# Block means of the first batch's values on TensorE instead of VectorE, and the fourth task's value products ahead of the next scores

## What is computed

```python
block, window = (32, 16)
k_sum = k.reshape(B, H, nb, block, D).max(axis=3)
v_sum = v.reshape(B, H, nb, block, D).mean(axis=3)
scores_l = scale * np.matmul(q, k.transpose(0, 1, 3, 2))      # kept where |i - j| < window
scores_s = scale * np.einsum('bhsd,bhnd->bhsn', q, k_sum) + np.log(block)
a = softmax(concatenate([scores_l_masked, scores_s]))
out = np.matmul(a, concatenate([v, v_sum]))
```

## Time and profile before

| | |
|---|---|
| time, median of 3 runs | 730.56 us (728.78 to 730.85) |
| the profiled execution | 730.36 us, its span 728.6 us |
| mean granted TensorE clock | 0.992 |
| busy: PE, DVE, ACT, POOL | 704.6, 404.5, 281.3, 66.8 us |
| DMA | 139.36 MB, mean 191 GB/s |

### The profile page before, as it was taken

One profiled execution on the slowest core, in us unless ns is written; L12 is line 12 of the kernel. 1 busy time (PEld: TensorE's weight loads), 2 busy tenths in 40 slices (PEclk: granted clock), 3 DMA queues, 4 the chain that ended last, 5 costly groups with the idle time before them and its releaser, 6 DMA issues.

```text
span 728.6 us, 12342 instructions
## 1 busy us (share of the span) xinstructions
PE 704.6 (97%) x4499; PEld 580.9 (80%) x4500; DVE 404.5 (56%) x1042; ACT 281.3 (39%) x653; POOL 66.8 (9%) x97
## 2 busy tenths in 40 slices
PE   5699999999999999999999999999999999899997
PEld 5578898898989889988988998899899884444444
DVE  4987584552795684754756364466447217453441
ACT  3745364451345433631621451064036113342430
POOL 2612000000000000000000000100100003323221
PEclk9999999999999999999999999999999999999999
DMA  9885632120708817613976739124530996699900
GB/s 206 217 196 117 133 82 55 41 48 4 286 5 326 331 60 287 285 64 103 417 301 276 261 115 367 51 103 186 219 115 10 377 348 232 243 393 396 370 3 22
DMA packets 92384, 139.36 MB, mean 191 GB/s; under 512 B 55172, under 2 KB 55456, under 8 KB 90656
## 3 DMA queue, kind: packets, MB, share of 16 engines
q1 hardware_dynamic: 89664, 133.89, 52.9%
q0 software_dynamic: 2656, 4.66, 1.9%
HBM read 104.05 MB, written 34.98 MB: 191 GB/s over the span
## 4 chain that ended last, share of the span: by engine, by line
PE 91%; DVE 4%; issue 1%; DMA 1%; ACT 1%; POOL 0%; DVEq 0%; SPq 0%; POOLq 0%
PE ps L1727 15%; PE ps L1729 15%; PE ps L1728 15%; PE ps L1977 8%; PE ps L1978 8%; PE ps L1979 8%; PE ps L2088 6%; PE ps L2116 6%; PE ps L1789 2%; PE ps L1761 2%; PE ps L1920 1%; PE ps L1775 1%; PE ps L2101 1%; PE ps L1740 1%; PE ps L1909 1%
## 5 line engine op out<-in xcount | busy, mean ns | idle before, releaser
L1977 PE MATMUL ps<-xt_hi,wb_hi 128*128 128x384 f32 x336 | 112.8, 336 | 0.0
L1979 PE MATMUL ps<-xt_hi,wb_lo 128*128 128x384 f32 x336 | 112.4, 334 | 0.0
L1978 PE MATMUL ps<-xt_lo,wb_hi 128*128 128x384 f32 x336 | 112.3, 334 | 0.0
L966 ACT ACTIVATE h_raw<-ps 128x384 f32<-128x384 f32 x96 | 47.1, 490 | 116.0 <-PE ps L1979 113.8
L1728 PE MATMUL ps<-v_lo_acc,hb_hi 128*128 128x512 f32 x216 | 84.2, 390 | 0.0
L1360 DVE SCALAR_TENSOR_TENSOR acc<-ps,dp,acc 128x512 f32<-128x512 f32 x36 | 27.0, 750 | 99.3 <-PE ps L1729 99.3
L1345 DVE TENSOR_TENSOR h_raw<-ps,h_raw 128x384 f32<-128x384 f32 x96 | 49.7, 552 | 44.4 <-PE ps L1979 44.3
L972 ACT ACTIVATE hb_hi<-h_raw 128x384 fp32r<-128x384 f32 x96 | 49.0, 525 | 52.5 <-DVE h_raw L1345 52.5
L1977 PEld LDWEIGHTS ps<-xt_hi,wb_hi 128*128 128x128 f32 x336 | 63.1, 188 | 0.4
L1978 PEld LDWEIGHTS ps<-xt_lo,wb_hi 128*128 128x128 f32 x336 | 63.1, 188 | 0.3
L1979 PEld LDWEIGHTS ps<-xt_hi,wb_lo 128*128 128x128 f32 x336 | 63.1, 188 | 0.0
(11 more groups left out here) (268 smaller groups left out, 1302.8 us busy)
## 6 DMA issues: line engine op xcount, KB each, us to landing
sets<-in_moe_w SPq DMA_DIRECT2D x72, 512.0 KB
w_aside<-wb_hi SPq DMA_DIRECT2D x3, 3584.0 KB, 17.0
w_aside<-wb_lo SPq DMA_DIRECT2D x3, 3584.0 KB, 24.8
wb_hi<-w_aside SPq DMA_DIRECT2D x21, 512.0 KB, 10.9
wb_lo<-w_aside SPq DMA_DIRECT2D x21, 512.0 KB, 11.7
acc<-in_moe_w SPq DMA_DIRECT2D x12, 768.0 KB, 5.2
w_raw<-in_moe_w SPq DMA_DIRECT2D x12, 512.0 KB, 5.5
stage<-in_k SPq DMA_DIRECT2D x16, 192.0 KB, 4.2
```

What stands on the lines that cost most here:

```text
L966: nc.scalar.activation(h_raw[:, f, half * GT:(half + 1) * GT], ps[:, bank, 0:GT], ACT.Copy).then_inc(put_by, 1)
L1977: mm(to, wb_hi[w], hi(c), start=(c == 0 and not onto), stop=False, skip_group_check=onto)
L1978: mm(to, wb_hi[w], lo(c), start=False, stop=False, skip_group_check=onto)
L1979: last = mm(to, wb_lo[w], hi(c), start=False, stop=(c == HALF_D - 1), skip_group_check=onto)
```

## The change

The four means of each block row of the first batch (`sum_values(0)` and `(1)` on DVE) are no longer made by additions. The values of the first batch are loaded in another layout (`load_early`: partition p holds positions 6p to 6p + 5 of each head, four DMAs of 192 KB in place of one of 768 KB) into the region of a later tensor, and PE multiplies six 128 x 32 matrices of 1/32 and 0 (`in_block`, made by POOL with a memset and two selections) with them (`block_means`, six products of 256 columns into 32 rows of PSUM bank 3). ACT copies the 24 x 256 means out (`copy_means`), and turn(a, 1), which writes the same bank, waits for that copy. The broadcasts of the lead tasks become one DMA each, with 128 numbers in a row. The pieces of the first weights no longer share a region with values of the first batch: POOL issues pieces 0 and 1 first, before any of the broadcasts, and 2 and 3 behind the broadcasts of tasks 0 and 1. pv(3) moves ahead of qk(4). The sums of c = 2, 3 stay on DVE.

```diff
             def load_values(c):
-                if c >= 2:
-                    sp.wait_ge(vsum_ok, 1 if c == 2 else c)
                 if c == 2:
                     sp.wait_ge(w1_ok, PIECES)
+                if c == 3:
+                    sp.wait_ge(vsum_ok, 1)
+            def load_early(c):
+                for h in range(4 * c, 4 * c + 4):
+                    sp.dma_start(v_early[:, h, :], vh[h].rearrange("(p t) d -> p (t d)", p=P)).then_inc(v_in[c], 16)
@@ SP's order
-            load_values(0)
+            load_early(0)
             load_windows(0)
...
-            load_values(1)
+            load_early(1)
@@ POOL
+            nc.gpsimd.memset(in_block[:, :, :], 1.0 / BLOCK).then_inc(s_const, 1)
+            for base, step, sign in ((0, SPAN, 1), (BLOCK - 1, -SPAN, -1)):
...
+                nc.gpsimd.affine_select(out=in_block[:, :, :], in_=in_block[:, :, :], compare_op=ALU.is_ge, fill=0.0, base=base,
...
             def first_w1(c):
-                if c:
-                    gp.wait_ge(vsum_ok, 2)
             def first_sums(a):
                 n = task(a)[2]
-                gp.wait_ge(vsum_ok, n // 2 + 1)
+                gp.wait_ge(means_ok, n // 2 + 1)
...
+                gp.dma_start(v_all[a % 2][WK:KW, :, :], means_of(n, slice(0, P))).then_inc(first_sums_in[a % 2], 16)
+            first_w1(0)
+            first_w1(1)
             first_sums(0)
             first_sums(1)
-            first_w1(0)
-            first_w1(1)
             first_w1(2)
             first_w1(3)
@@ ACT, lead(a)
                 exps(a + 1, 0)
+                if a < 2:
+                    copy_means(a)
                 evac_t(a, 0)
+            def copy_means(c):
+                rows = slice(NBP * c, NBP * c + NB)
+                act.wait_ge(means_ps, c + 1)
+                nc.scalar.activation(means[rows, :], ps[rows, 3, 0:4 * DH], ACT.Copy).then_inc(means_ok, 1)
@@ DVE
             norm(0, 0)
-            sum_values(0)
             lead(0)
-            sum_values(1)
             lead(1)
@@ PE, turn(a, h)
+                if a < 2 and h == 1:
+                    pe.wait_ge(means_ok, a + 1)
+            def block_means(c):
+                if c == 0:
+                    pe.wait_ge(s_const, 16)
+                else:
+                    pe.wait_ge(pt_ready, 2)
+                pe.wait_ge(v_in[c], 16 * 4)
+                for t in range(SPAN):
+                    last = mm(ps[NBP * c:NBP * (c + 1), 3, 0:4 * DH], in_block[:, t, :], v_early[:, 4 * c:4 * c + 4, t * DH:(t + 1) * DH],
+                              start=(t == 0), stop=(t == SPAN - 1))
+                last.then_inc(means_ps, 1)
@@ PE, lead(a)
                     transpose_queries(a + 2)
+                if a < 2:
+                    block_means(a)
                 if a:
                     pv(a - 1)
@@ PE, end of the lead
             turn(LEAD - 1, 1)
+            pv(LEAD - 1)
             qk(LEAD)
-            pv(LEAD - 1)
```

More of the change, by code:

```diff
@@ L170, in sparse_attention_moe_moe @@
             h_raw = sb_plain("h_raw", [P, FC, S])
-            sb_plain("under_v2_hi", [P, 4, D])
+            under_v2_hi = sb_plain("under_v2_hi", [P, 4, D])
             w_raw = sb_plain("w_raw", [P, BLOCKS, HALF_D, HALF_F])
@@ L214, in sparse_attention_moe_moe @@
         o += 2 * PS
-        v_sum = s1[:, o:o + VT * DH].rearrange("p (c d) -> p c d", c=VT)
-        o += VT * DH
+        v_sum = s1[:, o:o + VT // B * DH].rearrange("p (c d) -> p c d", c=VT // B)
+        o += VT // B * DH
         with ExitStack() as again:
@@ L222, in sparse_attention_moe_moe @@
         o = NT // 2 * D
-        v_rows = [a1[:, o:o + BLOCK * DH], a1[:, PIECE:PIECE + BLOCK * DH]]
+        v_rows = a1[:, o:o + BLOCK * DH]
         o += BLOCK * DH
         v_all = [v_first, a1[:, o:o + UH * P].rearrange("p (u c) -> p u c", u=UH)]
+        SPAN = S // P
+        NBP = 32
+        v_early = h_raw[:, 2:6, :].rearrange("p f (j c) -> p (f j) c", j=2)
+        in_block = under_v2_hi[:, 0, 0:SPAN * NBP].rearrange("p (t n) -> p t n", t=SPAN)
+        means = h_rows[0:2 * NBP, UH * KW:UH * KW + 4 * DH]
         k_sum = sb("k_sum", [P, NB])
@@ L288, in early_w1, with means_of @@
         def early_w1(c):
-            return early[:, c, :] if c < EARLY else v_rows[0][:, 0:PIECE]
+            return early[:, c, :] if c < EARLY else v_rows[:, 0:PIECE]
         def early_w2(c):
             return early[:, (c + 1) % EARLY, :]
-        def rows_of_values(c):
-            return v_rows[1 if c == 1 else 0]
+        def means_of(n, cols):
+            rows = NBP * (n // 2)
+            pair = means[rows:rows + NB, n % 2 * P:(n % 2 + 1) * P]
+            return pair[:, cols].rearrange("p (o d) -> p o d", o=1).broadcast_to((NB, UH, cols.stop - cols.start))
         def bank_x(k):
@@ L385, in sparse_attention_moe_moe @@
         vsum_step, vsum_ok = sem("vsum_step"), sem("vsum_ok")
+        means_ps, means_ok = sem("means_ps"), sem("means_ok")
         scores, masked, exped, sums_ok, inv_ok, normed = (
@@ L471, in load_sums @@
                 b, s, n = task(a)
-                c = b * PAIRS // 2 + n // 2
+                if b == 0:
+                    for h in range(2):
+                        sp.dma_start(v_all[a % 2][WK:KW, :, h * DH:(h + 1) * DH], means_of(n, slice(h * DH, (h + 1) * DH))).then_inc(sums_in[a % 2], 16)
+                    return
+                c = n // 2
                 sp.wait_ge(vsum_ok, c + 1)
@@ L715, in _ @@
             gp.wait_ge(s_const, made)
+            nc.gpsimd.memset(in_block[:, :, :], 1.0 / BLOCK).then_inc(s_const, 1)
+            made += 1
+            for base, step, sign in ((0, SPAN, 1), (BLOCK - 1, -SPAN, -1)):
+                gp.wait_ge(s_const, made)
+                nc.gpsimd.affine_select(out=in_block[:, :, :], in_=in_block[:, :, :], compare_op=ALU.is_ge, fill=0.0, base=base,
+                                        pattern=[[sign, SPAN], [-sign * BLOCK, NBP]], channel_multiplier=step).then_inc(s_const, 1)
+                made += 1
+            gp.wait_ge(s_const, made)
             def first_w1(c):
-                if c:
-                    gp.wait_ge(vsum_ok, 2)
                 gp.dma_start(early_w1(c), w1[0][c * P:(c + 1) * P, :]).then_inc(first_w1_in[c], 16)
@@ L1143, in sum_values @@
             def sum_values(c):
-                rows = rows_of_values(c)
-                dve.wait_ge(v_in[c % 2], 16 * (c // 2) + 16)
+                rows, k = v_rows, c - 2
+                dve.wait_ge(v_in[k], 16 * 4 + 16)
                 left = BLOCK * DH
@@ L1148, in sum_values @@
                     left //= 2
-                    if j or c:
-                        dve.wait_ge(vsum_step, STEPS * c + j)
+                    if j or k:
+                        dve.wait_ge(vsum_step, STEPS * k + j)
                     TT(rows[0:VR, 0:left], rows[0:VR, 0:left], rows[0:VR, left:2 * left], ALU.add).then_inc(vsum_step, 1)
-                dve.wait_ge(vsum_step, STEPS * c + STEPS)
-                nc.vector.tensor_scalar(v_sum[0:VR, c, :], rows[0:VR, 0:DH], 1.0 / BLOCK, None, ALU.mult).then_inc(vsum_ok, 1)
+                dve.wait_ge(vsum_step, STEPS * k + STEPS)
+                nc.vector.tensor_scalar(v_sum[0:VR, k, :], rows[0:VR, 0:DH], 1.0 / BLOCK, None, ALU.mult).then_inc(vsum_ok, 1)
             def lead(a):
@@ L1534, in _ @@
             add_rows(c, 0, c, 2, True)
-            dve.wait_ge(s_const, 15)
+            dve.wait_ge(s_const, 18)
             link(nc.vector.tensor_scalar(cnt_i[:, 0:1], side_first[:, :], -(QT - 1) / 2.0, 1.0 / QT, ALU.add, ALU.mult))
@@ L1781, in pv @@
                 if a < LEAD:
-                    pe.wait_ge(first_sums_in[a % 2], 16 * 2 * (a // 2 + 1))
+                    pe.wait_ge(first_sums_in[a % 2], 16 * (a // 2 + 1))
                 else:
@@ L1961, in _ @@
             pe.wait_ge(wg_in, 32)
-            pe.wait_ge(s_const, 15)
+            pe.wait_ge(s_const, 18)
             def block(t, j, i, moving, bank, onto=False):
```

2 lines of the change are left out of this document (1 added, 1 removed).

## The result

The changed kernel has a median of 731.52 us (729.15 to 732.61, 7 runs) against 729.16 us (727.73 to 730.85, 7 runs) for the kernel before in the same comparison: ratio 1.0028, interval 1.0015 to 1.0042, so 2.0 us slower. The forecast was 729.3 in 726.8 to 731.9, a change within 0.3% the likeliest. Both held, by little; the sign did not: 1.3 us were to be won, and 2.0 are lost.

What follows compares the result with a forecast made beforehand. PE, busy 704.6 of 728.6 us, bounds the kernel, so only the lead before about 50 us counts. 730.36 us of the profiled execution less 1.3 gives 729.1; the median, 0.2 above, is 729.3, range 726.8 to 731.9.

Steps and rivals of the forecast that it cites:

- mask(1, 0) near 16.9: In the lead, without the first sum on DVE, this mask starts near 16.9 and not 18.53, 1.6 us earlier.
- The removal of DVE's sums: In the lead, at most 6.2 us; at turn(2, 0) nothing of them is left and the change is 0.5 us behind.
- block_means(0) is hidden: The first set of six products falls into PE's idle time, 2.12 us before 20.13, so little of it is seen.
- low_o(3) no longer waits: Late in the lead, with pv(3) ahead of qk(4), low_o(3) no longer waits 0.49 us for it.
- The DMAs: In the lead, early weight pieces delay keys 3 by 1.5 us and queries 3 by 1.8: transposes at 24.9 and 26.5.
- rival C: Early pieces starve SP's loads; queries 3 beyond 26.5 delay everything behind one for one: 730 to 731, at worst 733; chance 0.12.
- block_means: Six products on PE take 0.7 to 1.4 us, taken as 1.3; the second set is on the path.
- what comes back: Behind turn(2, 0), three small gains bring mask(4, 0) to 43.0 from 44.05 and turn(4, 1) forward by 1.3 us.
- one of the two collisions: Tiny DVE instructions slowed by POOL's roundings cost 0.7 and 1.2 us; one such collision was expected to go, 0.9 us.
- The 0.5 us of the reorder: Late in the lead, moving pv(3) ahead of qk(4) gains 0.5 us, as PE has slack there.
- rival B: Spare transposes and ACT set the lead's pace, so the change gains too little: 730.0 to 731.0; chance 0.15.
- a clock that stays low: Sign that the forecast is wrong: the clock stays low for several stretches of the lead; no size given.

Runs made afterwards that it cites:

- e4: Changed kernel with block products cut by head into 24 of 64 columns, in four groups of 32 array columns; 730.69 us, ratio 1.0021 to the kernel before.
- e3: Changed kernel with all four pieces of the first weights behind the broadcasts of tasks 0 and 1 on POOL; 728.85 us, ratio 0.9989 to the kernel before.
- e5: Changed kernel with POOL's rounding of the fourth weight piece ahead of its broadcast for task 3; 729.57 us, ratio 1.0020 to the kernel before.
- e12: Changed kernel with late weight pieces, products in four groups, filler transposes in three places, and spares 4 and 4 instead of 12 and 12; 727.3 us, ratio 0.9973.
- e2: Kernel before with only the order of pv(3) and qk(4) changed; 729.09 us, ratio 1.0004.
- e14: Kernel before with 16 constant transposes ahead of turn(3, 0) and pv(3) ahead of qk(4); 727.9 us, ratio 0.9975.
- e10: Kernel before with 16 constant transposes ahead of turn(3, 0); 727.4 us, ratio 0.9971.
- e8: Changed kernel with 16 constant transposes ahead of turn(3, 0); 729.38 us, ratio 1.0011 to the kernel before.
- e9: Changed kernel with late weight pieces, products in four groups, and 8, 12 and 8 filler transposes in three places; 730.3 us, ratio 1.0008 to the kernel before.
- e13: Changed kernel with late weight pieces and filler transposes in three places, products as in the change; 727.5 us, ratio 0.9970 to the kernel before.
- e15: Changed kernel with early weight pieces as in the change, products in four groups, and filler transposes in three places; 732.13 us, ratio 1.0037 to the kernel before.

## Why the prediction was right and where it failed

**What held.** PE is full from 50 to 600 us, and the lead alone decides. mask(1, 0) near 16.9: 16.80. The removal of DVE's sums leaves nothing, because others stand behind: at 21.51 turn(0, 1) waits for ACT's copy, at 25.53 keys 3 are late. block_means(0) is hidden: with 0.88 us in place of 2.78 turn(0, 1) is at 21.42 instead of 21.51 (`e4`). low_o(3) no longer waits. The DMAs: queries 3 at 26.5 was forecast and 26.51 is measured, keys 3 at 24.9 and they come at 25.53. `e3` shows that the early pieces do it. The sizes were right; that the time would be lost in SP's issuing calls and not on the way to landing was not foreseen. This is rival C's mechanism, and the time lies where C put it (730 to 733), but C's own condition, queries 3 beyond 26.5, was not met. The trace agrees here with the Trainium skill's section that the prediction named (DMA: Bandwidth & Descriptors, Issuing engines are not separate DMA queues): loads from POOL delay those from SP, keys 3 by 1.5 us (25.53 against 24.05).

**A term that was mis-sized: block_means.** "Six are 0.7 to 1.4 us. I take 1.3" became 2.78. The row was misread. "x32" in the earlier trace rows counts recorded instructions, and each float32 product is recorded as two: the twelve added ones show as x24 in all, qk's twelve as x24 (a transpose is recorded once). The row thus holds 16 products, not 32. If they run side by side in pairs, as the prediction supposed, that is 0.23 each and 0.46 for a lone one, and six are 2.8. The Trainium skill (FP8 and Floating Point Precision, TensorE Precision Notes) had it right with its four passes: by the estimate in the prediction 2.6 for six, and 730.6 in all. The prediction set a row against the rule, and it was the reading of the row that was wrong. With queries 3 on time, turn(1, 1) is at 30.54 (29.1 forecast) and turn(2, 0) at 32.23 (30.9): 1.3 us late of the forecast.

But this isn't what turned the sign. `e4` is the test: its products take 0.88 us, less than the 1.3 that was assumed, turn(2, 0) comes at 31.27, near the forecast's 30.9, and the milestone is still at 216.02, the ratio at 1.0021. By the table the products leave 0.2 to 0.5 us at the milestone, the early pieces 1.3 to 1.5. The prediction had these in its sum as 1.5 to 1.8 us at keys and queries 3, and then let "what comes back" pay for them.

**The step that failed: what comes back.** From turn(2, 0) to turn(4, 1) the kernel before takes 18.60 us (30.43 to 49.03). The forecast has 16.8 (30.9 to 47.7), so 1.8 us come back; measured are 18.44 (32.23 to 50.67), so 0.2 do. (1) "I expect one of the two collisions to go, 0.9 us": one went and the other grew from 1.38 to 1.53, on the norm for which turn(3, 0) waits. `e5` and `e12` show that such a collision moves when the chain moves. (2) The 0.5 us of the reorder: `e2`, and `e14` against `e10` (212.79 and 212.51, medians 727.9 and 727.4), find nothing. (3) The clock, which the sum left out. "Half clock in 38 to 41.5 us as now" was named as an edge case of rival B, and a clock that stays low as a sign of being wrong. It became the case, and nearly twice as long: half clock from 38.8 to 45.4 and mask(4, 0) at 45.23, not 43.0. `e8` puts its price at 1.45 us. In the two versions of the changed kernel whose clock stays full behind turn(2, 0) the stretch has the length of the forecast: 16.65 us in `e8`, with norm(3, 0)'s collision still there, and 16.42 in `e5`. So it is the half clock that kept the stretch long in this execution. But the kernel before takes 16.78 us for it as soon as its clock stays full (`e10`), so that length is not owed to the change. In `e9`, `e13` and `e15`, which reach turn(2, 0) earlier, the stretch is 17.3 to 18.4 us even at the full clock, as other waits take over. The half clock isn't a cost that only the change has, for the kernel before has it too; and it hid what the experiments on the length of the products had won.

Together: forecast for turn(4, 1) 49.03 - 1.3 = 47.7, measured 50.67. Of the 3.0 us between them 1.3 are already there at turn(2, 0), by the products; the rest, 1.6, is what did not come back.

**Luck.** That 731.52 lies in the range is owed to the base. The forecast was worked out from a median of 730.56 (three runs); in the comparison the kernel before has 729.16, 1.4 us less. From that base the same sum gives 727.9 in 725.4 to 730.5, and the measured time lies outside.

**Open.** What sets the dip near 629 us; how often the lead's half clock comes in unprofiled executions, and with it how the 2.0 us of the medians divide; what SP's issuing calls wait for; and whether roundings placed for the shorter chain would let it arrive.

## What to carry to other kernels

Before a row is turned into a price, count the products in the code against the "x" of the row. A load that is moved to an earlier time with a DMA share near 1 is not free: look at who is issued next, and at how long its issuing calls take. A gain that other engines are to bring PE is only there if PE's clock is: put the granted clock into the sum. Work taken off an engine in a chain that crosses engines is worth only what the next one in the queue allows; here the chain ran into another engine's port, a late load and a halved clock, and a filler in PE's idle place gave 0.3% where the rewrite gave none.

## What the runs showed of the hardware

A multiplication of 128 x 360 on DVE took 3.10 us (`e12`) instead of 0.53 (`e10`) while POOL made two roundings of about 1 us, and an instruction on 128 x 3 numbers 1.53 instead of 0.16. With two loads of 512 KB issued early from POOL, two issuing calls on SP took 5.48 us instead of 1.77 (`e3`). The granted clock fell to half after PE had stood idle from 36 to 38 us and was half from 38.8 to 45.4; sixteen transposes, 1.91 us in all, in that idle place kept it at full (`e8`). Four groups of 32 columns with float32 products took 0.88 us instead of 2.78, 3.2 times faster; the Trainium skill (TensorEngine Tiling (Array Packing), Theoretical Speedup) names up to four for so narrow an output.
